# One attention loop on TensorE, a score mask built on the chip, and constants loaded in two parts

## The chip, the core and the metric

The kernel runs on one core of a Trainium2 chip. The metric is device time in microseconds (us). A core has five engines with instruction streams of their own: TensorE (PE, matmuls; its weight loads are listed as PEld), VectorE (DVE), ScalarE (ACT), GpSimd (POOL) and SyncE (SP, here the issuer of most DMAs). They meet only at semaphores.

## What is computed

Three stages, one after another: a decayed linear attention, a mixture of experts that sends each token to one of 8 experts, and a gated product with an output projection.

```python
def _attn_ref(q, k, v):                 # (4, 8, 768, 64) each
    gamma = 1.0 - 2.0 ** (-5.0 - np.arange(H))
    for t in range(S):
        state = gamma * state + einsum('bhd,bhe->bhde', k[:, :, t], v[:, :, t])
        y[:, :, t] = scale * einsum('bhd,bhde->bhe', q[:, :, t], state)

def _moe_ref(x, modality_id, w_gate, modality_bias, w1, w2):   # x: 3072 rows of 512
    logits = x @ w_gate + modality_bias[modality_id]
    e_idx = argmax(logits); gate_w = softmax(logits)[e_idx]
    out[mask] = gate_w[mask] * (relu(x[mask] @ w1[e]) @ w2[e])  # mask: rows of expert e

def _moe2_ref(x, w1, w2, w3, w_out):
    return ((x @ w1) * (x @ w2) @ w3) @ w_out
```

## The kernel before

The attention is cut into units: 6 chunks `c` of 128 positions by 4 batches `b`, 24 units in all, `u = 4c + b`. The state of a batch is carried from one chunk to the next, so unit `u` uses the state of unit `u - 4`. All four computing engines write their units out one after another in straight code (`each_unit`); there is no scheduler, so the order is the order in which the lines stand.

On PE a unit (`unit` in `block.tensor`) is five steps: `scores(u+1)`, the products of keys and queries of the *next* unit into banks 2 and 3; `from_state(u)`, what the old state contributes, into `attn`; `rows_and_logits(u-1)`, which turns the finished unit before into rows and multiplies by `w_gate`, into `pair`; `from_chunk(u)`, the masked scores by V, into `attn`; `update(u)`, the new keys by values, into banks 0 and 1. Chunk 0 has no `from_state` and chunk 5 no `update`. In the profile these are L749, L771, L762, L780 and L792.

The other engines follow. DVE, per unit: `masked(u)` multiplies the scores by the mask table `maskt` into `prob` (L981, two instructions); `keep_logits(u-2)` reduces the logits of two units ago out of `pair` (L987); `new_state(u-2)` (L999); `qdecay(u)`, which writes `qdk`, the decayed queries that `from_state(u)` reads (L991); in late units also a piece of weight preparation (L962). ACT, per unit and in this order: `keep(u-1)`, which waits for `s_lg`, that is for `keep_logits(u-1)`, and copies the rows out of `pair` to `x_keep`; then, after `from_chunk(u)`, the copy of `attn` to `xTu`, which signals `s_xTu` (both are L560, told apart by their tiles). POOL makes `kdk` for unit `u+2` when `update(u)` is done (L507). SP loads q, k transposed, v and k of each unit, 256 KB each, four units ahead, and stores `x_keep`.

`from_state(u)` waits for the copy of unit `u-1`, since both use `attn`; `scores(u+1)` waits for `masked(u)`, since banks 2 and 3 exist once; `rows_and_logits(u)` waits for `keep(u-1)`, since `pair` exists once.

At the start the mask table (512 KB) is SP's second transfer, and the table of small constants `small` (422 KB) is ACT's second. Behind the attention PE goes on with a product of `w3` and `w_out`, then with the experts' windows, then with the last stage, whose groups of 512 rows it already runs in an engine loop: `pe.Fori(1, NG - 1)`, four passes of one group.

Of the kernel before, what the change touches and what calls it, by code (L numbers as in the profile page):

```python
# [32 lines left out]
def build(nc, q_t, k_t, k, v, mod_id, w_gate, mod_bias, we1, we2, wa, wb, w3_t, w_out, out):  # L33
# [30 lines left out]
    lag = pos[None, :] - pos[:, None]  # L64
    mask_np = np.where(lag[:, None, :] >= 0, scale * gamma[None, :, None] ** np.maximum(lag, 0)[:, None, :], 0.0)
    half_head = lambda pair: gamma[2 * pair + (np.arange(P) // D)]
# [12 lines left out]
    c_mask = const("c_mask", mask_np.reshape(P, HP, 2, P).transpose(0, 2, 1, 3).reshape(P, H * P))  # L79
    c_qdec = const("c_qdec", qdec_np.reshape(P, HP * P))  # L80
    small_np = [("ident", np.eye(P)), ("before", before_np), ("ones", np.ones((P, P))), ("kdec", kdec_np.reshape(P, C * H)),
                ("grow", grow_np.reshape(P, C * HP)), ("segment", segment_np.reshape(P, E * NT)),
                ("erank", every(E - np.arange(E))), ("eidx", every(np.arange(E))),
# [14 lines left out]
    with ctx:  # L98
# [17 lines left out]
        sm = {n: small[:, a:a + w] for n, (a, w) in small_at.items()}  # L116
        ident = sm["ident"]
        iw = fixed("iw", [P, KD, XW])
        logits = fixed("logits", [P, E, NT])
# [29 lines left out]
        qdect = r("qdect", [P, HP, P])  # L149
        xTu = r("xTu", [P, KD, P])  # L150

# [31 lines left out]
        in_lane = r("in_lane", [P, NT, P])  # L183
        in_tile = r("in_tile", [P, NT, 2, NX])

        w_out_p = region(at_w + 32 * KB)("w_out_p", [P, 2, KF, DM], F32R)
# [45 lines left out]
        s_ldv = [sem(f"s_ldv{b}") for b in range(B)]  # L232
        s_mask = sem("s_mask")
        s_qk = sem("s_qk")
# [159 lines left out]
        def _(sp):  # L394
# [4 lines left out]
            def load(c, b, u):  # L399
                if c:  # L400
                    sp.wait_ge(s_up, u - B + 1)
                sp.dma_start(qkv[:, b, QT, :], slot_v[QT][b, c, :, :]).then_inc(s_ldq[b], 16)  # L402
                if u:
                    sp.dma_start(qkv[:, b, KT, :], slot_v[KT][b, c, :, :]).then_inc(s_ldq[b], 16)
                else:
                    sp.dma_start(maskt[:, :, :, :], c_mask.rearrange("p (r j t) -> p r j t", r=2, j=HP)).then_inc(s_mask, 16)
# [148 lines left out]
        def _(act):  # L555
            act.dma_start(qkv[:, 0, KT, :], slot_v[KT][0, 0, :, :]).then_inc(s_ldq[0], 16)
            act.dma_start(small[:, :], c_small).then_inc(s_const, 16)
            act.wait_ge(s_zero, 1)
            act.dma_start(iw[:, :, P:XW], w_gate.rearrange("(c p) e -> p c e", p=P)).then_inc(s_gatew, 16)
            copy = lambda o, i, **kw: act.activation(o, i, ACT.Copy, **kw)  # L560
# [19 lines left out]
            def unit(c, b, u):  # L580

                if u:
                    keep(u - 1)
                act.wait_ge(s_yTu, u + 1)
                copy(xTu[:, :, :], attn[:, :, 0:2 * P].rearrange("p r (m t) -> p r m t", m=2)).then_inc(s_xTu, 1)
# [7 lines left out]
            act.dma_start(mbias[:, :, :], mod_bias.unsqueeze(0).to_broadcast([P, NMOD, E])).then_inc(s_mod, 16)  # L593
            act.dma_start(mod_i[:, :, :], mod_id.bitcast(I32).rearrange("p (n two) -> p n two", two=2)).then_inc(s_mod, 16)
            each_unit(unit)
# [135 lines left out]
        def _(pe):  # L731
# [8 lines left out]

            def scores(c, b, u):
                pe.wait_ge(s_ldq[b], 32 * (c + 1))
# [9 lines left out]

            def rows_and_logits(u):
                pe.wait_ge(s_xTu, u + 1)
                if u:
                    pe.wait_ge(s_keep, u)
                else:
                    pe.wait_ge(s_gatew, 16)
                    pe.wait_ge(s_ident, KD)
                for j in range(KD):  # L760
                    for a in range(2):
                        i = pe.matmul(pair[halves(a), j, 0:XW], xTu[:, j, halves(a)], iw[:, j, :], start=True, stop=True, skip_group_check=True)  # L762
                i.then_inc(s_xl, 1)

            def from_state(b, u):
                pe.wait_ge(s_xTu, u)
                pe.wait_ge(s_qdk, u - B + 1)
                pe.wait_ge(s_state, u - B + 1)
                for j in range(HP):
# [4 lines left out]
            def from_chunk(c, b, u, first):  # L774
                pe.wait_ge(s_ldv[b], 16 * (c + 1))
                pe.wait_ge(s_prob, u + 1)
                for j in range(HP):
                    for r in range(2):
                        h = 2 * j + r
                        i = pe.matmul(attn[out_rows(j, r), r, j // 2 * P:(j // 2 + 1) * P], qkv[:, b, V, h * D:(h + 1) * D], prob[:, u % 2, r, j, :],  # L780
                                      start=(first and j < 2), stop=(j >= HP - 2), skip_group_check=True)
# [13 lines left out]

            def unit(c, b, u):
                if u + 1 < NT:
                    scores(c + (b + 1) // B, (b + 1) % B, u + 1)
                if c:
                    from_state(b, u)  # L800
                if u:
# [5 lines left out]
            scores(0, 0, 0)  # L807
            each_unit(unit)


# [14 lines left out]
            def counts():  # L825

                pe.wait_ge(s_const, 16)
                pe.wait_ge(s_one, 1)
                pe.wait_ge(s_keep, NT)
# [3 lines left out]

            w3_product(0, {2: lambda: rows_and_logits(NT - 1)})

# [103 lines left out]
        def _(dve):  # L939
# [61 lines left out]
            def unit(c, b, u):  # L1001
# [4 lines left out]
                if 1 < u <= NT - B + 1:  # L1006
                    if u == 2:
                        dve.wait_ge(s_const, 16)
                    new_state((u - 2) // B, (u - 2) % B, u - 2)
# [292 lines left out]
```

## Time and profile before

| | us |
|---|---|
| median of 3 runs (897.7 to 898.63) | 897.8 |
| the profiled execution | 897.12 |
| its span, first to last instruction | 895.4 |
| PE busy in it | 855.5 (96%) |
| DVE, ACT, POOL busy | 286.3, 238.5, 87.2 |

The profiled execution is 1.72 us longer than its span, and 0.68 us under the median. PE's share of busy time is an average over all stages: the attention takes roughly the first 112 us, and there PE has gaps that the later stages do not have. In the views below, "idle before" is the time an engine stood still before an instruction, with what ended it; "issue" means that the profile shows nothing that it waited for. PE's single-precision matmuls of the attention are listed as two passes each, so the eight matmuls of a step appear as x16 and the sixteen of `scores` as x32.

### The profile page before, as it was taken

To read this page: it belongs to the slowest core of one execution; us is meant where nothing else is said; L and a number is where in the kernel's file an instruction comes from. 1 tells how busy PE (TensorE), PEld (TensorE's weight loads), DVE (VectorE), ACT (ScalarE), POOL (GpSimd) and SP (SyncE) were. 2 spreads that over 40 slices of the span, in tenths; PEclk is the share of its full clock that TensorE was granted. 3 is DMA by queue.
4 is the path that set the end of the run, shared out by engine and by line. 5 is a ranking of instruction groups with operands and counts; after the bars stand their busy time and mean duration, and the time that the engine had idled before them with its cause. 6 is when DMAs were issued, how large, how long until landed. Compare 5 with 4: busy or idle time off the path is not lost.

```text
span 895.4 us, 14636 instructions
## 1 busy us (share of the span) xinstructions
PE 855.5 (96%) x5812; PEld 737.4 (82%) x5813; DVE 286.3 (32%) x495; ACT 238.5 (27%) x388; POOL 87.2 (10%) x110
## 2 busy tenths in 40 slices
PE   6989999998979999999998999999999999999995
PEld 5878878787979998888888788888888888888884
DVE  2658588531212334121416331221220230230210
ACT  1223423421212333121326322222231221231210
POOL 2222002202011020202000001001001001001001
PEclk9999999999999999999999999999999999999999
DMA  9999951323031252203054102002002002001000
GB/s 326 368 352 335 303 215 48 141 95 96 5 91 31 63 188 94 94 0 94 0 187 142 47 1 83 12 1 82 12 0 94 0 0 94 0 0 48 0 13 35
DMA packets 43484, 84.81 MB, mean 95 GB/s; under 512 B 7728, under 2 KB 7728, under 8 KB 43440
## 3 DMA queue, kind: packets, MB, share of 16 engines
q1 hardware_dynamic: 33376, 60.33, 19.6%
q0 software_dynamic: 4736, 14.72, 5.2%
q10 hardware_dynamic: 5328, 9.13, 3.1%
q8 instruction: 33, 0.54, 0.3%
q14 instruction: 11, 0.09, 0.0%
HBM read 63.16 MB, written 21.00 MB: 94 GB/s over the span
## 4 chain that ended last, share of the span: by engine, by line
PE 91%; issue 2%; DVE 2%; DMA 1%; SPq 1%; ACT 1%; ACTq 0%; POOL 0%; DVEq 0%
PE bank L387 47%; PE attn L387 33%; PE pair L762 3%; PE bank L749 2%; PE attn L780 2%; PE pair L842 1%; DMA qkv<-in_k_t_dram 1%; PE attn L771 1%; PE bank L792 1%; PE bank L894 1%; DVE we_p L962 0%; DVE w3T L962 0%; ACTq L342 0%; ACT we_p L560 0%; SPq L402 0%
## 5 line engine op out<-in xcount | busy, mean ns | idle before, releaser
L387 PE MATMUL bank<-yT,wab 128*128 128x512 f32 x1152 | 262.2, 389 | 1.7 <-issue 1.7
L387 PEld LDWEIGHTS bank<-yT,wab 128*128 128x128 f32 x1152 | 216.1, 188 | 46.7 <-issue 1.9
L387 PE MATMUL bank<-xT,we_p 128*128 128x512 f32 (+2 forms) x768 | 155.3, 364 | 11.5 <-issue 7.9
L387 PEld LDWEIGHTS bank<-xT,we_p 128*128 128x128 f32 x768 | 138.1, 195 | 28.3 <-issue 10.4
L387 PE MATMUL attn<-hT,we_p 128*128 128x512 f32 (+2 forms) x768 | 153.6, 357 | 0.0
L387 PEld LDWEIGHTS attn<-hT,we_p 128*128 128x128 f32 x768 | 132.9, 188 | 14.6
L387 PE MATMUL attn<-wc,gT 128*128 128x512 f32 x576 | 131.5, 389 | 0.0
L387 PEld LDWEIGHTS attn<-wc,gT 128*128 128x128 f32 x576 | 108.1, 188 | 22.5
L1242 DVE TENSOR_TENSOR g<-bank,acopy 128x512 f32<-128x512 f32 x48 | 33.2, 692 | 258.8 <-PE bank L387 258.8
L1203 DVE SCALAR_TENSOR_TENSOR hT<-bank,hT 128x512 fp32r<-128x512 f32 x64 | 44.1, 691 | 172.4 <-ACT hT L633 172.4
L633 ACT ACTIVATE hT<-bank 128x512 fp32r<-128x512 f32 x64 | 38.2, 598 | 114.9 <-PE bank L387 114.9
L560 ACT ACTIVATE gT<-g 128x512 fp32r<-128x512 f32 x48 | 30.3, 632 | 136.6 <-DVE g L1242 136.6
L548 POOL DMA_INDIRECT out_dram<-otile,row_id x24 | 23.2, 968 | 377.8 <-ACT otile L560 377.8
L560 ACT ACTIVATE yout<-attn 128x512 f32<-128x512 f32 x32 | 19.1, 597 | 114.6 <-PE attn L387 114.6
L560 ACT ACTIVATE acopy<-bank 128x512 f32<-128x512 f32 x48 | 28.7, 598 | 67.3 <-PE bank L387 67.3
L962 DVE TENSOR_TENSOR gT<-g,gT 128x512 fp32r<-128x512 f32 x48 | 33.3, 693 | 33.8 <-ACT gT L560 33.8
L560 ACT ACTIVATE otile<-attn,meta_in 128x512 f32<-128x512 f32 x24 | 16.6, 690 | 100.0 <-PE attn L387 100.0
L981 DVE TENSOR_TENSOR prob<-bank,maskt 128x512 f32<-128x512 f32 x48 | 30.8, 683 | 27.8 <-PE bank L749 21.1
L749 PE MATMUL bank<-qkv 64*64 64x128 f32 x768 | 28.4, 288 | 8.7 <-DMA qkv<-in_q_t_dram 4.4
L962 DVE TENSOR_TENSOR xT<-pair,xT 128x512 fp32r<-128x512 f32 x30 | 19.3, 686 | 54.1 <-ACT xT L560 53.9
L524 POOL DMA_INDIRECT xin<-x_rows,x_id x32 | 31.0, 969 | 11.1 <-issue 7.3
L560 ACT ACTIVATE x_keep<-pair 128x512 f32<-128x512 f32 x24 | 14.3, 598 | 63.6 <-DVE logits L987 63.6
(148 smaller groups left out, 559.7 us busy)
## 6 DMA issues: line engine op xcount, KB each, us to landing
we_raw<-in_moe_w_dram SPq DMA_DIRECT2D x6, 2048.0 KB, 9.1
yT_sorted<-yout ACTq DMA_DIRECT2D x8, 1024.0 KB, 4.9
qkv<-in_q_t_dram SPq DMA_DIRECT2D x24, 256.0 KB, 4.0
qkv<-in_v_dram SPq DMA_DIRECT2D x24, 256.0 KB, 6.0
x_rows<-x_keep SPq DMA_DIRECT2D x24, 256.0 KB, 5.7
ytile<-yT_sorted SPq DMA_DIRECT2D x6, 1024.0 KB, 5.1
qkv<-in_k_t_dram SPq DMA_DIRECT2D x23, 256.0 KB, 5.8
qkv<-in_k_dram SPq DMA_DIRECT2D x20, 256.0 KB, 6.5
```

The costliest lines, as they stand in the source:

```text
L387: i = pe.matmul(out_, left(a), right(b), start=(first and n == 0), stop=(last and n == 2), **kw)
L524: pool.indirect_dma_start(xin[:, t, :], None, x_rows[:, :], bass.IndirectOffsetOnAxis(ap=x_id[:, t:t + 1], axis=0)).then_inc(s_xin, 16)
L548: pool.indirect_dma_start(out[:, :], bass.IndirectOffsetOnAxis(ap=row_id[:, n:n + 1], axis=0), otile[:, n % 2, :], None).then_inc(s_out[n ...
L560: copy = lambda o, i, **kw: act.activation(o, i, ACT.Copy, **kw)
L633: act.activation(hT[:, HI, f, :], bank[f % 2][:, :], ACT.Relu).then_inc(s_hhi, 1)
L749: i = pe.matmul(bank[2 + r][halves(a), j * P:(j + 1) * P], qkv[head_rows(r), b, KT, keys], qkv[head_rows(r), b, QT, j * P:(j + 1) * P], st ...
L762: i = pe.matmul(pair[halves(a), j, 0:XW], xTu[:, j, halves(a)], iw[:, j, :], start=True, stop=True, skip_group_check=True)
L780: i = pe.matmul(attn[out_rows(j, r), r, j // 2 * P:(j // 2 + 1) * P], qkv[:, b, V, h * D:(h + 1) * D], prob[:, u % 2, r, j, :], start=(fir ...
L962: tt(pair(LO), raw, pair(HI).bitcast(F32), ALU.subtract).then_inc(sm_, 1)
L981: i = tt(prob[:, u % 2, r, :, :], bank[2 + r][:, :].rearrange("p (j t) -> p j t", j=HP), maskt[:, r, :, :], ALU.mult)
L1203: dve.scalar_tensor_tensor(hT[:, LO, f, :], bank[f % 2][:, :], 0.0, hT[:, HI, f, :].bitcast(F32), ALU.max, ALU.subtract).then_inc(s_hlo, 1)
L1242: tt(g32[:, f % 2, :], bank[2 + f % 2][:, :], acopy[:, f % 2, :], ALU.mult).then_inc(s_g, 1)
```

## The change

Five things change. PE's units of chunks 1 to 4 become one engine loop of four units that runs four times; chunks 0 and 5 stay as straight code. Inside a unit `from_chunk(u)` now stands ahead of `rows_and_logits(u-1)`, and `from_state`'s three waits (`s_xTu`, `s_qdk`, `s_state`) now stand ahead of `scores(u+1)`; `xTu` gets two buffers, since `rows_and_logits(u-1)` now runs while the copy of unit `u` may be due. The mask table is no longer loaded: PE multiplies a column of powers by a row of powers (`rank1`, 8 KB), and DVE multiplies the products by a triangle of ones. `small` is loaded in two parts: the identity, the strict triangle and `kdec` early, from ACT, the rest from SP with unit 1. The modality tables are issued in ACT's unit 2, the query table `qdect` with SP's unit 2, and `w_gate` comes laid out in one piece per partition. The orders of `unit` on DVE, ACT and POOL are the same as before, apart from those loads.

```diff
-                    sp.dma_start(maskt[:, :, :, :], c_mask...).then_inc(s_mask, 16)
...
                 if u == 1:
+                    sp.dma_start(small[:, first_w:], c_small[:, first_w:]).then_inc(s_rest, 16)
+                if u == 2:
                     sp.dma_start(qdect[:, :, :], c_qdec...).then_inc(s_tables, 16)
...
-            act.dma_start(small[:, :], c_small).then_inc(s_const, 16)
+            act.dma_start(rank1[:, :, :, :], c_rank1...).then_inc(s_rank1, 16)
+            act.dma_start(small[:, 0:first_w], c_small[:, 0:first_w]).then_inc(s_const, 16)
+            act.dma_start(iw[:, :, P:XW], w_gate...).then_inc(s_gatew, 16)
             act.wait_ge(s_zero, 1)
-            act.dma_start(iw[:, :, P:XW], w_gate...).then_inc(s_gatew, 16)
...
             def unit(c, b, u):      # ACT
+                if u == 2:
+                    act.dma_start(mbias[:, :, :], mod_bias...).then_inc(s_mod, 16)
+                    act.dma_start(mod_i[:, :, :], mod_id...).then_inc(s_mod, 16)
                 if u:
                     keep(u - 1)
                 act.wait_ge(s_yTu, u + 1)
-                copy(xTu[:, :, :], attn...).then_inc(s_xTu, 1)
+                copy(xTu[:, u % 2, :, :], attn...).then_inc(s_xTu, 1)
...
+            def mask_products():
+                pe.wait_ge(s_rank1, 16)
+                for r in range(2):
+                    for j in range(HP):
+                        h = 2 * j + r
+                        i = pe.matmul(bank[6 + r][:, j * P:(j + 1) * P], rank1[0:1, 0, h, :], rank1[0:1, 1, h, :], start=True, stop=True)
+                i.then_inc(s_outer, 1)
+
+            def scores(c, b, u, first=False, state_of=None):
+                pe.wait_ge(s_ldq[b], c * 32 + 32)
+                if not first:
                     pe.wait_ge(s_prob, u)
+                if state_of is not None:
+                    pe.wait_ge(s_xTu, u - 1)
+                    pe.wait_ge(s_qdk, state_of + 1)
+                    pe.wait_ge(s_state, state_of + 1)
+                pe.sem_inc(s_begun, 1)
...
-            def unit(c, b, u):
-                if u + 1 < NT:
-                    scores(c + (b + 1) // B, (b + 1) % B, u + 1)
-                if c:
-                    from_state(b, u)
-                if u:
-                    rows_and_logits(u - 1)
-                from_chunk(c, b, u, c == 0)
-                if c < C - 1:
-                    update(b, u, c == 0)
+            def unit(c, b, u, first=False, last=False):
+                if not (last and b == B - 1):
+                    scores(c + (b + 1) // B, (b + 1) % B, u + 1, state_of=None if first else (c - 1) * B + b)
+                elif last:
+                    pe.wait_ge(s_xTu, u)
...
+                if not first:
+                    from_state(b)
+                elif b:
+                    pe.wait_ge(s_xTu, u)
+                from_chunk(c, b, u, first)
+                if not (first and b == 0):
+                    rows_and_logits((b - 1) % B, u - 1, first and b == 1)
+                if not last:
+                    update(b, u, first)
...
+            mask_products()
+            scores(0, 0, 0, True)
+            for b in range(B):
+                unit(0, b, b, first=True)
+            with pe.Fori(0, C - 2) as past:
+                for b in range(B):
+                    unit(past + 1, b, past * B + (B + b))
+            for b in range(B):
+                unit(C - 1, b, (C - 1) * B + b, last=True)
...
-            dve.wait_ge(s_mask, 16)
+            dve.wait_ge(s_const, 16)
+            link(tt(tri[:, :], sm["before"], ident, ALU.add))
+            dve.wait_ge(s_outer, 1)
+            for r in range(2):
+                link(tt(maskt[:, r, :, :], bank[6 + r]..., tri..., ALU.mult))
             each_unit(unit)
```

On PE, one whole unit of chunk 1 in the kernel before, from `scores` to `update`, with the semaphores that each first matmul waits for:

```order
L749 MATMUL bank<-qkv 64x128 [waits s_prob,s_ldq2]
L749 MATMUL bank<-qkv 64x128 x15
L771 MATMUL attn<-qdk,state 64x128 [waits s_state,s_qdk,s_xTu]
L771 MATMUL attn<-qdk,state 64x128 x7
L762 MATMUL pair<-iw,xTu 64x136 [waits s_keep,s_xTu]
L762 MATMUL pair<-iw,xTu 64x136 x7
L780 MATMUL attn<-prob,qkv 64x128 [waits s_prob,s_ldv1]
L780 MATMUL attn<-prob,qkv 64x128 x7
L792 MATMUL bank<-qkv,kdk 64x64 [waits s_state,s_kdk]
L792 MATMUL bank<-qkv,kdk 64x64 x7
```

The wait for `s_xTu` of the finished unit stands behind `scores`. The same unit in the changed kernel, inside the loop (L770 is `scores`, L789 `from_state`, L798 `from_chunk`, L783 `rows_and_logits`, L810 `update`):

```order
L770 MATMUL bank<-qkv 64x128 [waits s_state,s_qdk,s_prob,s_xTu]
L770 MATMUL bank<-qkv 64x128 x15
L789 MATMUL attn<-qdk,state 64x128 x8
L798 MATMUL attn<-prob,qkv 64x128 [waits s_prob,s_ldv2]
L798 MATMUL attn<-prob,qkv 64x128 x7
L783 MATMUL pair<-iw,xTu 64x136 [waits s_keep,s_xTu]
L783 MATMUL pair<-iw,xTu 64x136 x7
L810 MATMUL bank<-qkv,kdk 64x64 [waits s_state,s_kdk]
L810 MATMUL bank<-qkv,kdk 64x64 x7
```

Three waits moved from `from_state` to `scores`, and the products into `pair` moved behind those of `prob`. On ACT the units stand as they did; this is its start in the changed kernel, up to the second unit:

```order
L562 DMA qkv<-in_k_t_dram 128x512
L563 DMA rank_102<-c_rank 1x2048
L564 DMA small<-c_small 128x304
L565 DMA iw<-in_moe_w_gate_dram 128x4x8
L567 ACT_TABLE_LOAD
L567 ACTIVATE act_warm<-zero 128x1 [waits s_zero]
L567 ACTIVATE xTu<-attn 128x512 [waits s_yTu]
L567 ACTIVATE x_keep<-pair 128x512 [waits s_lg]
L567 ACTIVATE xTu<-attn 128x512 [waits s_yTu]
L590 DMA mbias<-in_moe_modality_bias_dram 128x16
L591 DMA mod_i<-in_moe_modality_id_dram 128x48
```

The two modality loads moved from ahead of the first copy to behind the second; `x_keep` of a unit still stands ahead of `xTu` of the next.

## Rows read from the trace of the kernel before

**Rows 1.** Busy time by stretch: us, PE, PEld, DVE, ACT, POOL, clock, DMA share, GB/s

```profile
0.00:10.00 10.00, 1.98 (x32) 1.59 (x33) 1.31 (x3) 1.50 (x3) 2.33 (x10) 1.00 0.80 272
10.00:20.00 10.00, 9.29 (x184) 8.34 (x186) 3.33 (x7) 1.71 (x3) 2.20 (x3) 1.00 1.00 365
...
30.00:40.00 10.00, 8.02 (x184) 7.16 (x178) 6.08 (x16) 2.20 (x4) 2.08 (x2) 1.00 1.05 388
```

**Rows 2.** Chain that ended last, in order: start us, us, what; attention and its end

```profile
7.96 10.50 DMA qkv<-in_k_t_dram
18.51 1.10 PE bank L749 x32
...
22.03 1.03 PE bank L749 x32
...
25.48 1.17 PE bank L749 x32
...
30.75 1.04 issue
...
53.75 2.00 issue
...
99.24 1.03 PE bank L749 x32
...
102.66 1.03 PE bank L749 x32
...
110.15 1.58 PE bank L387 x6
111.74 1.10 PE pair L762 x16
```

**Rows 3.** Timeline of PE, one regular unit: start us, busy us, engine, line, instruction

```profile
91.86 1.10 PE L749 MATMUL bank<-qkv 64*64 64x128 f32 x32
...
92.79 0.62 PE L771 MATMUL attn<-qdk,state 64*64 64x128 f32 x16
...
93.34 1.15 PE L762 MATMUL pair<-iw,xTu 128*64 128x136 f32 x16
...
94.31 1.04 PE L780 MATMUL attn<-prob,qkv 128*64 128x128 f32 x16
...
95.19 0.64 PE L792 MATMUL bank<-qkv,kdk 128*64 128x64 f32 x16
...
95.75 1.10 PE L749 MATMUL bank<-qkv 64*64 64x128 f32 x32
```

**Rows 4.** Timeline, from rows_and_logits through DVE and ACT to PE; idle and releaser in brackets

```profile
106.89 0.60 ACT L560 ACTIVATE xTu<-attn 128x512 f32<-128x512 f32 x1
...
107.54 0.67 PE L771 MATMUL attn<-qdk,state 64*64 64x128 f32 x16 [0.70 <-ACT xTu L560]
...
108.13 1.15 PE L762 MATMUL pair<-iw,xTu 128*64 128x136 f32 x16
...
109.33 0.19 DVE L987 TENSOR_REDUCE logits<-pair 128x8 f32<-128x32 f32 x1 [0.60 <-PE pair L762]
109.55 0.60 ACT L560 ACTIVATE x_keep<-pair 128x512 f32<-128x512 f32 x1 [1.55 <-DVE logits L987]
```

**Rows 5.** Timeline of DVE, ACT and POOL in one regular unit

```profile
73.63 0.18 DVE L987 TENSOR_REDUCE logits<-pair 128x8 f32<-128x32 f32 x1
...
73.84 0.60 ACT L560 ACTIVATE x_keep<-pair 128x512 f32<-128x512 f32 x1 [2.28 <-DVE logits L987]
...
74.06 0.68 DVE L991 TENSOR_TENSOR qdk<-qkv,qdect 128x512 f32<-128x512 f32 x1
74.33 0.59 ACT L560 ACTIVATE xTu<-attn 128x512 f32<-128x512 f32 x1
```

**Rows 6.** Timeline of POOL and DVE where they overlap

```profile
67.03 1.04 POOL L507 TENSOR_TENSOR kdk<-qkv,small 128x512 f32<-128x512 f32 x1 [2.85 <-PE bank L792]
67.61 1.01 DVE L962 TENSOR_TENSOR w_out_p<-w_out_raw,w_out_p 128x512 fp32r<-128x512 f32 x1 [0.91 <-ACT w_out_p L560]
```

**Rows 7.** Timeline of the start

```profile
6.80 1.29 DVE L981 TENSOR_TENSOR prob<-bank,maskt 128x512 f32<-128x512 f32 x2 [6.68 <-DMA maskt<-c_mask]
7.26 1.00 POOL L498 COPY iw<-small 128x128 f32<-128x128 f32 x4 [6.31 <-DMA small<-c_small]
10.20 1.99 PE L749 MATMUL bank<-qkv 64*64 64x128 f32 x32 [3.79 <-DMA qkv<-in_k_t_dram]
```

**Rows 8.** Costliest groups, the loop of the last stage (busy, mean ns, idle before, releaser)

```profile
L387 PE MATMUL bank<-yT,wab 128*128 128x512 f32 x1152 | 262.2, 389 | 1.7 <-issue 1.7
```

**Rows 9.** Waits of PE from 200 to 260 us: total us, times, longest

```profile
PE bank L387 <- issue: 7.9, 2, 4.9
```

More of the change, by code:

```diff
@@ L64, in build @@
     lag = pos[None, :] - pos[:, None]
-    mask_np = np.where(lag[:, None, :] >= 0, scale * gamma[None, :, None] ** np.maximum(lag, 0)[:, None, :], 0.0)
+    rank1_np = np.stack([gamma[:, None] ** -pos[None, :], scale * gamma[:, None] ** pos[None, :]])
     half_head = lambda pair: gamma[2 * pair + (np.arange(P) // D)]
@@ L149, in build @@
         qdect = r("qdect", [P, HP, P])
-        xTu = r("xTu", [P, KD, P])
+        xTu = r("xTu", [P, 2, KD, P])
+        tri = r("tri", [P, P])
         x_keep = region(at_i)("x_keep", [P, NT, DM])
@@ L232, in build @@
         s_ldv = [sem(f"s_ldv{b}") for b in range(B)]
-        s_mask = sem("s_mask")
+        s_rank1 = sem("s_rank1")
+        s_outer = sem("s_outer")
+        s_rest = sem("s_rest")
+        s_begun = sem("s_begun")
         s_qk = sem("s_qk")
@@ L580, in unit @@
             def unit(c, b, u):
+                if u == 2:
+                    act.dma_start(mbias[:, :, :], mod_bias.unsqueeze(0).to_broadcast([P, NMOD, E])).then_inc(s_mod, 16)
+                    act.dma_start(mod_i[:, :, :], mod_id.bitcast(I32).rearrange("p (n two) -> p n two", two=2)).then_inc(s_mod, 16)
                 if u:
@@ L584, in unit @@
                 act.wait_ge(s_yTu, u + 1)
-                copy(xTu[:, :, :], attn[:, :, 0:2 * P].rearrange("p r (m t) -> p r m t", m=2)).then_inc(s_xTu, 1)
+                copy(xTu[:, u % 2, :, :], attn[:, :, 0:2 * P].rearrange("p r (m t) -> p r m t", m=2)).then_inc(s_xTu, 1)
                 if side_piece(u) is not None:
@@ L751, in scores, with rows_and_logits @@
                 i.then_inc(s_qk, 1)
-            def rows_and_logits(u):
+            def rows_and_logits(b, u, first=False):
                 pe.wait_ge(s_xTu, u + 1)
-                if u:
+                if not first:
                     pe.wait_ge(s_keep, u)
@@ L761, in rows_and_logits, with from_state @@
                     for a in range(2):
-                        i = pe.matmul(pair[halves(a), j, 0:XW], xTu[:, j, halves(a)], iw[:, j, :], start=True, stop=True, skip_group_check=True)
+                        i = pe.matmul(pair[halves(a), j, 0:XW], xTu[:, b % 2, j, halves(a)], iw[:, j, :], start=True, stop=True, skip_group_check=True)
                 i.then_inc(s_xl, 1)
[L765 to L768, printed above, removed]
+            def from_state(b):
                 for j in range(HP):
@@ L794, in update @@
                 i.then_inc(s_up, 1)
-            def unit(c, b, u):
-                if u + 1 < NT:
-                    scores(c + (b + 1) // B, (b + 1) % B, u + 1)
-                if c:
-                    from_state(b, u)
-                if u:
-                    rows_and_logits(u - 1)
-                from_chunk(c, b, u, c == 0)
-                if c < C - 1:
-                    update(b, u, c == 0)
-            scores(0, 0, 0)
-            each_unit(unit)
+            def unit(c, b, u, first=False, last=False):
[3 more added lines that the diff above has]
+                    pe.wait_ge(s_xTu, u)
+                    pe.wait_ge(s_qdk, (c - 1) * B + b + 1)
+                    pe.wait_ge(s_state, (c - 1) * B + b + 1)
+                if not first:
+                    from_state(b)
[15 more added lines that the diff above has]
+                unit(C - 1, b, (C - 1) * B + b, last=True)
             def w3_product(f, amid={}):
@@ L832, in counts @@
                 pe.matmul(bank[7][:, 0:E * NT], sm["ones"], chosen, start=True, stop=True).then_inc(s_cnt, 1)
-            w3_product(0, {2: lambda: rows_and_logits(NT - 1)})
+            w3_product(0, {2: lambda: rows_and_logits(B - 1, NT - 1)})
             def x_rows(w, chunks):
@@ L1283 @@
     swapped = place.reshape(-1)
-    laid["moe_w_gate"] = inputs["moe_w_gate"][swapped]
+    laid["moe_w_gate"] = inputs["moe_w_gate"][swapped].reshape(4, 128, -1).transpose(1, 0, 2).reshape(128, -1)
     laid["moe_w1"] = inputs["moe_w1"][:, swapped]
```

25 lines of the change are left out of this document (12 added, 13 removed).

## The prediction

> **What bounds the kernel now.** I read the busy time by stretch first, then the chain that ended last, then single units in the timeline. PE carries almost the whole span, so the question for each edit is whether PE waits more or less. In the attention it has gaps: 8.02 us busy in the ten from 30 to 40 [rows 1]. From the scores of unit 4 at 22.03 to those of unit 23 at 102.66 the chain runs for 80.63 us over 19 units [rows 2]. A regular unit takes 95.75 - 91.86 = 3.89 us, its five steps back to back [rows 3]; one without an update 102.66 - 99.24 = 3.42, the one of chunk 0 25.48 - 22.03 = 3.45 [rows 2]. So 16 x 3.89 + 2 x 3.42 + 3.45 = 72.5 us are PE's own work, and 8.1 us are gaps: five pieces called issue (the first and the longest in [rows 2]), with small gaps beside them. Ahead of that the start is set by transfers: the scores of unit 3, at 18.51, come 0.05 us after a K load that landed at 18.46 [rows 2].
>
> **The loop's gain.** If PE finds the loop's code in place on passes two to four, most of the 8.1 us go. Chunk 0, the first pass and chunk 5 still run code that PE meets for the first time, so I leave 1.0 us of gaps (bounds 0, and 3.1 for three pieces like the first). Loop-backs fall between an update and the scores, where PE will be waiting anyway (next part). Term: -8.1 + 1.0 = -7.1 us.
>
> The Trainium skill speaks against the loop in "Runtime: NRT & Kernel Launch", section "Instruction fetch mechanics": code is fetched ahead in sequence, and a taken branch to a target outside the window held forces a fetch, so unrolled code is preferred. The trace has a loop of this kind, the last stage's four passes of one group, and all its first products together stand idle for 1.7 us by issue [rows 8], so the row does not bear the rule out; by the row the sum stays, by the rule it becomes the third rival below.
>
> **The order and the moved waits: the largest term.** In the changed unit `scores(u+1)` waits for the copy `xTu(u-1)`. ACT's order is unchanged: ahead of that copy stands `keep(u-2)`, which waits for DVE's `keep_logits(u-2)`, which waits for `rows_and_logits(u-2)`. That step used to stand ahead of `from_chunk`, so its two followers were done by the time `from_chunk` ended. Now it stands behind it, so PE sends the products into `pair`, and what follows on DVE and ACT has only the update to hide behind. Let R be the start of `rows_and_logits`. From R to the logits' reduction 109.33 - 108.13 = 1.20 us, from there to `x_keep` 0.22 [rows 4], from `x_keep` to the copy behind it 74.33 - 73.84 = 0.49 [rows 5], from the copy's start to PE's first matmul 107.54 - 106.89 = 0.65 [rows 4]: 2.56 us from R to the next scores. From scores to R the steps keep their lengths in the new order: 92.79 - 91.86 = 0.93 for the scores, 0.55 for `from_state` (to the start at 93.34), 95.19 - 94.31 = 0.88 for `from_chunk` [rows 3]: 2.36 us. The unit therefore repeats every 2.36 + 2.56 = 4.92 us. No row shows what the five waits and the loop's register arithmetic ahead of `scores` add behind the last release. In the row with three such waits PE starts 0.05 us after the copy ends (106.89 + 0.60 to 107.54 [rows 4]), which lies in the 0.65; zero more is one bound, 0.35, seven times that, the other, and I take 0.08, near the row. So 5.0 us a unit, 1.11 over PE's work, in 16 units, and 1.58 over in the two without an update: 17.8 + 3.2 us. The first wait of the kind, ahead of the scores of unit 5, stands behind a unit without `from_state`: 0.93 + 0.96 + 2.56 = 4.45 for 3.45, 1.0 us more. Term: +22.0 us. Queued behind the waiting scores is all else of the unit; DVE's mask, SP's loads (after `update`) and POOL move with PE, so nothing of it is off the path.
>
> Behind the last scores nothing much changes: before, 111.74 - 102.66 = 9.08 us to the last `rows_and_logits` [rows 2]; after, 4.92 + 0.55 + 0.88 + 2.56 = 8.9, with six products in between as before. Term: -0.1 us.
>
> DVE could set the period instead of ACT. `qdk` starts 74.06 - 73.63 = 0.43 us behind the reduction and takes 0.68 [rows 5], so it ends at R + 1.20 + 0.43 + 0.68 = R + 2.31, under 2.56. But POOL's `kdk` now starts close by: the update starts 0.97 us after R, by the spacing of `rows_and_logits` to the next step, lasts 0.64 [rows 3], and POOL some 0.15 us later (an estimate from the regular units), R + 1.76, against R + 1.63 for `qdk`. Where POOL was first in this trace, DVE's product of two SBUF tiles took 1.01 us and ended 0.55 us after POOL did [rows 6]. Here DVE is first by 0.13 us, so I add nothing; the other order is a rival.
>
> The Trainium skill, "SBUF — State Buffer", section "Who interferes with whom", calls this an exclusive lock for the whole instruction, held by whichever starts first. The 1.01 us agree, and by that rule too DVE keeps its 0.68 us and the sum stays.
>
> **Start.** 512 KB of mask go from SP's queue ahead of the K load of unit 3; the rest of `small` and `qdect` still stand ahead of it. At 365 GB/s [rows 1] this is 1.4 us, at 272 GB/s 1.9; with the smaller `w_gate` pieces I take -1.5 us (bounds 0, where something else is as late, and -3.0, where the second part of `small` also slips behind). The mask costs PE 16 small passes, no more than an update's 0.64 us [rows 3], and DVE three operations, two of them like a mask product of 0.65 [rows 7]. Its inputs land before 7.26, when the whole of `small` had [rows 7], by some 2 us since they are 152 of 422 KB; the first mask product then starts near 7, as before at 6.80, and the scores that wait for it stood until 10.20 for a load [rows 7]. If that cover goes, up to 1 us is lost there, and the load of unit 3 hides it again. The two modality loads put about 1.2 us of issue on ACT in unit 2; `keep(1)` and `xTu(2)` are queued behind, and ACT idles 2.28 us before a regular `keep` [rows 5], so I cost them at nothing.
>
> **Sum.** -7.1 + 22.0 - 0.1 - 1.5 = +13.3 us. Against the profiled execution of 897.12 us this is 910.4; the median lies 0.68 above that execution, so the time I name is 911.0. What follows the attention moves with it.
>
> **Rivals.**
>
> *Faster: PE does not wait for the copy.* If something in the new order let `xTu` be ready when the update ends, a unit would stay at 3.89 us and the change would give 7.1 + 1.5 = 8.6 us: 889. The point from which it decides is the period: 18 units and the first must not pay more than 8.6 us, so 4.3 us a unit. For it speaks only that the second `xTu` buffer allows a copy while the rows are still being read; against it stands ACT's order, `keep` ahead of the copy, and four measured steps that sum to 2.56 us, where 1.53 (the update, 0.56 after 0.97) are covered. Chance 0.06, with 0.02 for a time within 0.2% (1.8 us, about what a measurement of this kernel can tell from no change).
>
> *POOL first.* If `kdk` takes the port before `qdk`, `qdk` ends at R + 1.76 + 1.04 + 0.55 = R + 3.35 and a unit takes 5.76 us, 0.76 more in 16 units: +12.2, so 923. The margin is 0.13 us. Chance 0.14.
>
> *Loop-backs fetch code.* PE's two entries into new branches cost 7.9 us, the longest 4.9, the other 3.0 [rows 9]. Three loop-backs at 3.0 to 4.9 us, less the 1.11 us of waiting that covers them: +5.7 to +11.4, so 917 to 922. Against it stands the 1.7 us of [rows 8]. Chance 0.06.
>
> *PE's clock falls.* The scores took 1.99 us at 10.20 [rows 7] and 1.10 later [rows 3], so at the lower of its two levels PE's 3.5 us of a period would grow by about 2.8, +50 in all: 961. PE would be busy 3.89 of 5.0 us, 78%; the stretch from 30 to 40 had 80% and a granted clock of 1.00 [rows 1]. Chance 0.04.
>
> **How the numbers follow.** The forecast has 0.68: its own ends are a period of 4.92 to 5.27 (-1.4, +4.9), gaps 0 to 3.1 (-1, +2.1) and a start of -3.0 to 0 (-1.5, +1.5), which do not all fall to one side: 907 to 918. The range adds the loop-backs, the near half of POOL first and some way down towards the gain: 905 to 922; out of it are the gain, the clock and half of POOL first, under 0.2. Faster 0.06, same 0.02, slower 0.92.
>
> **What would show it.** PE's waits should list `scores` on ACT's `xTu`, some 18 times, about 1.1 us each; scores should start 5.0 us apart; the issue pieces between 40 and 110 us should be gone; the mask's transfer too, and the first product of unit 3 should start near 17. `qdk` at 0.68 us says that DVE is first, at 1.5 that POOL is. Scores 3.9 us apart would prove the main term wrong.

## The result

The changed kernel takes 913.69 us (913.23 to 914.68, 4 runs) against 897.75 for the kernel before: a ratio of 1.0179, 95% interval 1.0161 to 1.0196. It is slower by 15.9 us; the forecast was 911.0 within 905 to 922, slower with a chance of 0.92.

The page of the changed kernel, its span and the busy times:

```profile
span 911.5 us, 14723 instructions
PE 857.0 (94%) x5828; PEld 738.9 (81%) x5829; DVE 289.2 (32%) x498; ACT 236.9 (26%) x388; POOL 91.7 (10%) x110
```

PE's busy time is almost the old one, so the time went into waiting. PE's waits in the first 150 us of the changed kernel (total us, times, longest):

```profile
PE bank L770 <- ACT xTu L567: 21.6, 19, 1.6
PE pair L754 <- DMA rank<-c_rank: 4.6, 1, 4.6
PE bank L770 <- issue: 1.8, 2, 1.5
PE attn L789 <- ACT xTu L567: 1.4, 1, 1.4
```

`scores` (L770) waits 19 times for ACT's copy, 1.1 us each. One unit of the changed kernel in the timeline shows the whole path, from `rows_and_logits` (L783) over the reduction (L1019), `x_keep` and `xTu` to the next scores:

```profile
56.16 1.10 PE L783 MATMUL pair<-iw,xTu 128*64 128x136 f32 x16
...
57.30 0.19 DVE L1019 TENSOR_REDUCE logits<-pair 128x8 f32<-128x32 f32 x1 [1.09 <-PE pair L783]
...
57.53 0.60 ACT L567 ACTIVATE x_keep<-pair 128x512 f32<-128x512 f32 x1 [4.11 <-DVE logits L1019]
57.74 0.68 DVE L1023 TENSOR_TENSOR qdk<-qkv,qdect 128x512 f32<-128x512 f32 x1
...
57.88 1.45 POOL L513 TENSOR_TENSOR kdk<-qkv,small 128x512 f32<-128x512 f32 x1 [3.75 <-PE bank L810]
58.02 0.59 ACT L567 ACTIVATE xTu<-attn 128x512 f32<-128x512 f32 x1
...
58.71 1.10 PE L770 MATMUL bank<-qkv 64*64 64x128 f32 x32 [0.99 <-ACT xTu L567]
```

From R = 56.16 to the scores it is 2.55 us; the sum made from [rows 4, 5] was 2.56. The pieces of the chain that ended last show how far the scores lie apart:

```profile
22.77 1.03 PE bank L770 x32
...
27.36 1.10 PE bank L770 x32
...
63.66 1.10 PE bank L770 x32
...
68.75 1.10 PE bank L770 x32
...
73.94 1.10 PE bank L770 x32
...
78.89 1.10 PE bank L770 x32
...
83.84 1.10 PE bank L770 x32
...
114.18 1.10 PE bank L770 x32
...
119.24 1.10 PE bank L770 x32
...
128.35 1.10 PE pair L783 x16
```

Inside a pass of the loop the distances are 5.09, 5.19, 4.95 and 4.95 us, 5.05 in the mean. The chain has 0.23 and 0.33 us by issue between the copy and the scores in the first two units of a pass and 0.09 in the other two; that the first two compute their wait values behind the release of the copy and the others ahead of it is a guess, since the profile does not list register instructions. The straight units of chunk 5, which have no such arithmetic, have 0.20 us there and lie 5.06 us apart, so on the whole the loop costs nothing here. The mean from unit 5 to unit 23 is (119.24 - 27.36) / 18 = 5.10 us, against 3.89 for a regular unit before [rows 3].

### The profile page after: what moved, and what is told of

The parts are those of the page before. It is cut to its first block, busy times and chain, and to the rows that moved or that the text cites. A ratio compares the mean times of both kernels' runs of the same rounds, so it can differ in the third digit from the quotient of the medians.

```text
span 911.5 us, 14723 instructions
## 1 busy us (share of the span) xinstructions
PE 857.0 (94%) x5828; PEld 738.9 (81%) x5829; DVE 289.2 (32%) x498; ACT 236.9 (26%) x388; POOL 91.7 (10%) x110
## 3 DMA queue, kind: packets, MB, share of 16 engines
q1 hardware_dynamic: 33376, 60.08, 19.3%
## 4 chain that ended last, share of the span: by engine, by line
PE 89%; DVE 3%; ACT 3%; issue 3%; ACTq 0%; DMA 0%; POOL 0%; DVEq 0%
PE bank L393 45%; PE attn L393 32%; PE bank L770 3%; PE attn L798 3%; PE pair L783 2%; PE pair L874 1%; ACT x_keep L567 1%; ACT xTu L567 1%; PE attn L789 1%; PE bank L926 1%; DVE logits L1019 0%; DVE we_p L994 0%; PE pair L754 0%; DMA rank<-c_rank 0%; DVE w3T L994 0%
## 5 line engine op out<-in xcount | busy, mean ns | idle before, releaser
L393 PEld LDWEIGHTS bank<-xT,we_p 128*128 128x128 f32 x768 | 136.2, 191 | 29.7 <-issue 11.3
L770 PE MATMUL bank<-qkv 64*64 64x128 f32 x768 | 28.5, 287 | 23.4 <-ACT xTu L567 21.6
L770 PEld LDWEIGHTS bank<-qkv 64*64 64x64 f32 x768 | 22.8, 140 | 26.7 <-issue 26.5
L567 ACT ACTIVATE otile<-attn,meta_in 128x512 f32<-128x512 f32 x24 | 16.6, 690 | 100.0 <-PE attn L393 100.0
L994 DVE TENSOR_TENSOR xT<-pair,xT 128x512 fp32r<-128x512 f32 x30 | 19.3, 686 | 54.1 <-ACT xT L567 53.9
```

What stands on the lines that cost most here:

```text
L393: i = pe.matmul(out_, left(a), right(b), start=(first and n == 0), stop=(last and n == 2), **kw)
L770: i = pe.matmul(bank[2 + r][halves(a), j * P:(j + 1) * P], qkv[head_rows(r), b, KT, keys], qkv[head_rows(r), b, QT, j * P:(j + 1) * P], st ...
L994: tt(pair(LO), raw, pair(HI).bitcast(F32), ALU.subtract).then_inc(sm_, 1)
```

## Experiments

Theory 1, from the prediction: two chains follow `rows_and_logits` before the next scores, ACT's `keep` and copy (2.56 us) and DVE's `qdk` (2.31 us), and only the update covers them. Rivals: the loop itself is the loss, or ACT's order alone. Each set of runs had the kernel before run beside it, at 895.5 to 895.8 us there, so times of different sets are compared by their ratio to it. The times in the expectations go by the kernel before at 897.75 us, some 2 us more than in these sets.

### The copy ahead of the keep

```diff
             def unit(c, b, u):      # ACT
-                if u:
-                    keep(u - 1)
                 act.wait_ge(s_yTu, u + 1)
                 copy(xTu[:, u % 2, :, :], attn...).then_inc(s_xTu, 1)
+                if u:
+                    keep(u - 1)
```

> The changed kernel with one edit: ACT copies attn to xTu ahead of the keep of the unit before. Changed kernel 913.7 us, scores 5.10 us apart in the mean. Theory 1 (two followers of rows_and_logits stand between it and the next scores: ACT's keep and copy at R+2.56, and DVE's qdk at R+2.31, R being the start of rows_and_logits): the copy is now hidden, but the scores still wait for qdk, so the period falls only to about 4.8, 18 x 0.3 = 5 us: about 908. Theory 2 (the loop with its register arithmetic is the loss): nothing moves, 913.7. Theory 3 (ACT's order alone is the loss): period 3.9 to 4.0, about 893.

Measured: 910.49 us, ratio 1.0162 (1.0127 to 1.0198). PE's waits of this kernel in the first 150 us:

```profile
PE bank L770 <- DVE qdk L1023: 10.3, 11, 1.5
PE bank L770 <- issue: 9.4, 10, 1.5
```

ACT is gone from the list and DVE's `qdk` stands in its place. "issue" is here very probably the same wait, put down by the profile to nothing, since those scores start 0.21 us behind the end of `qdk` (57.88 behind 57.67, 62.74 behind 62.53), and 0.15 us where the profile names it (67.55 behind 67.40):

```profile
56.99 0.68 DVE L1023 TENSOR_TENSOR qdk<-qkv,qdect 128x512 f32<-128x512 f32 x1
...
57.88 1.10 PE L770 MATMUL bank<-qkv 64*64 64x128 f32 x32 [0.91 <-issue]
```

By its time this kernel cannot be told from the changed one (1.0162 for 1.0179, within the interval), so the time does not decide between the theories; the trace does. In passes 2 to 4 the scores lie 4.80 to 4.87 us apart, as theory 1 said. The attention ends 3.5 us earlier in the trace (its `w3` product begins at 123.22 for 126.76), a little under the 5 expected, since unit 7 and the late units gain less. ACT's order alone is not the cause; it is one of two chains of nearly one length.

### The three waits back at from_state

```diff
             def scores(c, b, u, first=False, state_of=None):
...
-                if state_of is not None:
-                    pe.wait_ge(s_xTu, u - 1)
-                    pe.wait_ge(s_qdk, state_of + 1)
-                    pe.wait_ge(s_state, state_of + 1)
...
+            def from_state(c, b, u):
+                pe.wait_ge(s_xTu, u)
+                pe.wait_ge(s_qdk, (c - 1) * B + b + 1)
+                pe.wait_ge(s_state, (c - 1) * B + b + 1)
+                pe.sem_inc(s_begun, 1)
```

> The changed kernel with from_state's three waits (xTu, qdk, state) moved back from scores to from_state, behind a semaphore increment like that of scores; ACT's order and PE's order of steps stay. Theory 1: the copy still comes at R+2.56, but PE now has update and scores to do until R+1.53+0.93 = 2.46, so only 0.1 to 0.35 us a unit are exposed: period 4.05 to 4.25, 895 to 898 us. Theory 2 (loop): about 913. Theory 3 (ACT's order alone): the copy is as late as before and from_state waits for it instead, 910 or more.

Measured: 901.59 us, ratio 1.0067 (1.0046 to 1.0089). The chain that ended last in this kernel, scores and a gap of the first pass:

```profile
31.64 1.94 issue
...
60.98 1.03 PE bank L766 x32
...
65.11 1.03 PE bank L766 x32
...
69.33 1.03 PE bank L766 x32
```

A unit takes 4.12 to 4.26 us, within what was expected. The time is 4 us above the expected 895 to 898, by ratio 6: two gaps of 1.94 and 1.90 us in the first pass, of the kind seen before [rows 2], are back, now that PE does not stand waiting where they fall; the rest was not followed.

### rows_and_logits back ahead of from_chunk

```diff
-                from_chunk(c, b, u, first)
                 if not (first and b == 0):
                     rows_and_logits((b - 1) % B, u - 1, first and b == 1)
+                from_chunk(c, b, u, first)
```

> The changed kernel with rows_and_logits put back ahead of from_chunk; the waits stay at scores, ACT's order stays. Theory 1: the keep is done by the time from_chunk ends, so behind from_chunk there is the copy alone, 0.06 + 0.60 + 0.05 and some 0.15 of register work, against an update of 0.56: 0.3 us exposed, period about 4.2, about 897 us. Theory 2 (loop): 913. Theory 3 (ACT's order): keep still stands ahead of the copy, so 910 or more.

Measured: 901.51 us, ratio 1.0062 (1.0042 to 1.0083). PE's waits of this kernel, and two pieces of its chain, the scores ten units apart:

```profile
PE bank L770 <- ACT xTu L567: 8.3, 19, 0.9
```

```profile
50.17 1.10 PE bank L770 x32
...
93.35 1.10 PE bank L770 x32
```

The copy is still the last to come, but by 8.3 us in all for 21.6; units take 4.24 to 4.49 us, mean (93.35 - 50.17) / 10 = 4.32, for some 4.2 expected. The time missed the expected 897 by 4.5 us: 0.12 a unit is some 2 of them, and the two units around DVE's preparation of the bias tables take 45.69 - 35.66 = 10.03 us, 1.4 over two others. ACT's order is that of the changed kernel in this run and in the one ahead of it, so the rival that it alone is the loss falls: each of PE's two edits costs little by itself, the order alone 0.3 us a unit over 3.89 (the run ahead of this one), the moved waits alone 0.4 (this run); together they cost 1.2.

### The loop written out

```diff
-            with pe.Fori(0, C - 2) as past:
-                for b in range(B):
-                    unit(past + 1, b, past * B + (B + b))
+            for c in range(1, C - 1):
+                for b in range(B):
+                    unit(c, b, c * B + b)
```

> The changed kernel with the loop of chunks 1 to 4 written out as straight code, all else the same. Theory 1: PE waits for the copy as before, period 5.06 as in the straight chunk 5 now, and code that is met for the first time adds gaps, part of which the waits hide: 913 to 919 us. Theory 2 (the loop is the loss, code in place the gain): the loss of some 22 us goes and the gaps of 8 come back: about 899.

Measured: 914.87 us, ratio 1.0217 (1.0194 to 1.024). PE's waits of this kernel:

```profile
PE bank L770 <- ACT xTu L567: 22.1, 19, 1.6
```

The waits are the same, so the loop is not the loss. And no gap by issue like those before (0.94 us and more) comes back although all code of the attention is straight again: its `w3` product begins at 126.97, for 126.76 with the loop. The scores lie 5.06 us apart here too. The trace also shows what the instruction queue that differs with PE's code (q8 in the DMA view) moved: nothing between 50 and 110 us with the loop, nine blocks of code, 0.02 MB each, without it. So in this order the loop saves nine fetches of code, which lie under the waits, and 0.2 us of the attention. By ratio the straight form is 0.4% slower (1.0217 for 1.0179); where that would lie the two traces, with spans of 911.8 and 911.5 us, do not show.

### What the loop is worth without the waits

Both PE edits undone, once with the loop and once as straight code; the mask is made on the chip in both:

```diff
-                from_chunk(c, b, u, first)
                 if not (first and b == 0):
                     rows_and_logits((b - 1) % B, u - 1, first and b == 1)
+                from_chunk(c, b, u, first)
...
-                    pe.wait_ge(s_xTu, u - 1)      # the three waits again at from_state
...
-            with pe.Fori(0, C - 2) as past:       # only in the straight form
+            for c in range(1, C - 1):
...
```

> The changed kernel with both PE edits undone inside the loop (rows_and_logits ahead of from_chunk, the three waits at from_state behind a semaphore increment), so the loop, the mask on the chip and the two-part constants remain. Theory 1 (order and waits are the whole loss): period 3.9 to 4.1, few gaps, the start 0.7 us later than before: 892 to 895 us against 897.75. Theory 2 (register arithmetic in the loop costs as much as it saves): 897 or more.

> As the kernel with both PE edits undone, but with chunks 1 to 4 as straight code: of the change there remain the mask on the chip and the constants. Theory 1: the kernel before with its gaps of 8 us and a start 0.7 us later, 898 to 899 us; its distance to the looped form is what the loop is worth without the waits, 3 to 6 us. Theory 2 (loop worth nothing): the same time as the looped form.

Measured: 895.86 us with the loop, ratio 0.9993 (0.9976 to 1.001); 903.11 as straight code, 1.0083 (1.0061 to 1.0105). The loop is worth 7.2 us here, more than the 3 to 6 expected, and both times lie above the expected ones (892 to 895, 898 to 899). In the chain of the looped form the units of passes 2 to 4 follow without a gap, and the product behind the attention begins at 108.86; in that of the straight form it begins at 114.31, so 5.4 of the 7.2 us lie in the attention:

```profile
51.96 1.03 PE bank L766 x32
...
55.85 1.03 PE bank L766 x32
...
59.74 1.03 PE bank L766 x32
...
108.86 1.58 PE bank L393 x6
```

```profile
26.19 1.41 issue
...
38.47 2.41 issue
...
62.51 1.48 issue
...
86.07 1.36 issue
...
114.31 1.59 PE bank L393 x6
```

The first fence is the looped form, the second the straight one. At 3.89 us a unit the register arithmetic of the loop does not show. From 50 to 100 us the instruction queue moved no block in the looped form and eight in the straight one, and each of the straight form's six gaps (the four shown, 0.75 at 32.74 and 0.82 at 79.57) begins within some 2 us behind such a block. That goes with fetching as their cause; it does not show why seven other blocks from 25 to 100 us brought no gap.

### The mask loaded again

The changed kernel with the mask from memory, and the looped form of the old PE order with it:

```diff
+                    sp.dma_start(maskt[:, :, :, :], c_mask...).then_inc(s_outer, 16)   # SP, second transfer
...
-            act.dma_start(rank1[:, :, :, :], c_rank1...).then_inc(s_rank1, 16)
...
-            mask_products()
...
-            link(tt(tri[:, :], sm["before"], ident, ALU.add))
-            dve.wait_ge(s_outer, 1)
-            for r in range(2):
-                link(tt(maskt[:, r, :, :], bank[6 + r]..., tri..., ALU.mult))
+            dve.wait_ge(s_outer, 16)
```

> The changed kernel with the mask table loaded again by SP as second transfer, without the products of powers on PE and their multiplication on DVE; constants still in two parts. Theory 1 (the start of the changed kernel is 2.2 us later than forecast because the mask's inputs land at 8.4 us and 16 passes of 0.24 us run ahead of the first scores): the mask lands near 6.8 as before, the scores of unit 4 start near 21.3 in place of 22.8, about 912.3 us. Rival (the start is set by the K loads in either form): the 512 KB come back ahead of them and nothing is gained, 913.7 or up to 915.

> As the kernel with both PE edits undone inside the loop, and the mask table loaded as before, so the loop and the two-part constants remain of the change. Theory 1: another 1.4 us less than with the mask made on the chip, 891 to 894 us. Rival for the start (K loads set it): the same as with the mask made on the chip, or up to 1 us more.

> The kernel of old PE order, loop and loaded mask, beside the shifted one on the same chip: 0.9916 of the kernel before as in its first run, about 7.5 us less.

Measured: 906.49 us, ratio 1.0113 (1.0092 to 1.0134), for the changed kernel with the loaded mask; 887.88, ratio 0.9916 (0.9893 to 0.9939), and in the second run 887.97, ratio 0.9902 (0.9882 to 0.9921), for the looped old order with it. The last is the one form faster than both kernels, by 0.8 to 1.0% than the one before.

The gain of some 6 us (1.0179 to 1.0113) is four times what was expected; in the old order it is 8.0 (895.86 to 887.88). The start of the changed kernel shows where the expected part lies:

```profile
4.59 3.78 PE L754 MATMUL pair<-rank 1*128 1x128 f32 x16 [4.59 <-DMA rank<-c_rank]
...
8.30 1.99 PE L770 MATMUL bank<-qkv 64*64 64x128 f32 x32
8.51 0.29 DVE L1056 TENSOR_TENSOR tri<-small 128x128 f32<-128x128 f32 x1 [8.38 <-DMA small<-c_small]
...
8.83 1.42 DVE L1059 TENSOR_TENSOR maskt<-pair,tri 128x512 f32<-128x512 f32 x2
...
10.42 1.29 DVE L1013 TENSOR_TENSOR prob<-bank,maskt 128x512 f32<-128x512 f32 x2 [0.17 <-PE bank L770]
11.81 1.99 PE L770 MATMUL bank<-qkv 64*64 64x128 f32 x32 [1.53 <-issue]
```

The products of powers take 3.78 us, 0.24 a pass, ahead of the first scores, and the first part of `small`, though it is a third of the table, lands at 8.5 us, behind the 7.26 of the whole table before [rows 7]. The second scores start at 11.81 for 10.20. With the loaded mask the scores of unit 4 start at 21.07 for 22.77, and the product behind the attention 1.9 us earlier. The other 4 us lie in the experts' stage, and the next experiment shows what most of them hang on.

### The code moved by 33 instructions

```diff
+            for _ in range(33):
+                pe.sem_inc(s_begun, 1)
             scores(0, 0, 0, True)
```

> The kernel of old PE order, loop and loaded mask with 33 semaphore increments on PE ahead of its first scores, where it waits 4.4 us for a load anyway; nobody waits on them. They stand where the 32 instructions of the mask's products stand in the changed kernel, so all later code lies at the place that it has there. Theory 1 (the gap of 5 us at the end of the experts' first window and the 1.4 us near 480 us hang on where the code lies): both come back, 6 us more than the same kernel without them. Rival (they hang on the mask's work or the transfers of the start): at most 1 us more.

Measured, on the looped old order with the loaded mask: 893.57 us, ratio 0.9976 (0.996 to 0.9992), 5.6 us more than the same kernel without the increments beside it. The chain of the shifted form at the experts' first window and at the end of it:

```profile
210.34 2.65 issue
248.32 4.43 issue
```

The unshifted form has one of the two, and in the other's place 0.29 us in its first run, shown here, and 0.20 in its second:

```profile
208.21 2.36 issue
245.92 0.29 issue
```

By its place, behind the 192 products of the first window, the second gap is where PE branches over code that it has not run. It stands in the kernel before too, with 4.87 us, and in the changed kernel with 5.12; in all, eleven of the thirteen kernels have it, with 4.2 to 5.2 us, and the two without it, the changed and the old order with the loop and the loaded mask and no increments, have 0.2 to 0.3 in three traces. The DMA view ties it to fetched code: in each of the eleven traces that instruction queue moved one block of 0.02 MB inside the gap, and in the three others none in the 5 us from the same place on. There the last block had come ahead of the branch (at about 247 for 249.34 in the second run of the unshifted form).

The gap costs more than its length: behind it the granted clock of the shifted form is 0.50, the lower of its two levels, from 252.8 to 254.8, and the next 96 products take 18.34 us; in the unshifted form beside it the clock is 1.00 there and they take 16.91. Together this is 5.7 us. The rest of the distance nearly cancels: with the increments the product behind the attention begins 1.4 us later (108.90 for 107.54), but the first window ends 1.0 earlier (248.32 for 249.34), since in that run of the unshifted form the first gap was the longer one (3.48 us), with a clock of 0.53 to 0.76 in the 4.6 us behind it.

So most of what the mask seemed to cost beyond the start is the place of later code, moved by the 32 instructions of its products: with the loaded mask the changed kernel has 0.30 for its 5.12 us. The gap of 1.4 us near 480 us did not come back, so that half of the expectation was wrong.

### POOL first

Two tries at the rival in which `kdk` takes the shared port ahead of `qdk`: one small DVE copy ahead of `qdk`, then three.

```diff
+                    for a in (tmax, tsum, gate):     # the first try: tmax alone
+                        dve.tensor_copy(a[:, :], sm["ones"][:, 0:NT])
                     qdecay(c, b)
```

> The changed kernel with one small DVE copy (128x24, some 0.17 us) ahead of qdk in chunks 1 to 5, so that POOL's kdk, at R+1.76, starts before qdk, at R+1.8, in place of behind it. If the two exclude each other and the first keeps the other out: qdk ends 0.55 us behind kdk, at R+3.35, the unit repeats every 5.75 us in the 16 units with a kdk, and the kernel takes about 924 us. If they only slow each other a little: qdk ends by R+2.6, ACT's copy stays the last to come, 914 us.

> As with one small DVE copy ahead of qdk, which moved it by 0.08 us only and left it 0.05 us ahead of POOL's kdk; now three copies into three tiles, so qdk comes near R+1.9, behind kdk's R+1.76. If the first keeps the other out: qdk ends near R+3.35, the 16 units with a kdk repeat every 5.7 us, scores wait for qdk instead of the copy, about 924 us. If they share: qdk ends by R+2.7, 0.15 us over the copy, 916 us at most.

The first try gave 914.44 us, ratio 1.0196 (1.0168 to 1.0224), and decided nothing: the copy ran into `qdk`'s start and delayed it by 0.08 us only, so DVE was still first by 0.05. The second gave 937.71, ratio 1.0462 (1.0442 to 1.0483). Its timeline:

```profile
70.81 1.10 POOL L513 TENSOR_TENSOR kdk<-qkv,small 128x512 f32<-128x512 f32 x1 [6.49 <-PE bank L810]
...
70.91 1.54 DVE L1023 TENSOR_TENSOR qdk<-qkv,qdect 128x512 f32<-128x512 f32 x1
...
72.66 1.10 PE L770 MATMUL bank<-qkv 64*64 64x128 f32 x32 [2.01 <-issue]
```

`qdk` starts 0.10 us behind `kdk`, takes 1.54 us instead of 0.68 and ends 0.54 after `kdk`, the 0.55 read from [rows 6]. The price was right; the time is 13.7 us above the 924 expected, mostly since a second rival came with it, the clock. The busy times of two stretches of this kernel, with the granted clock ahead of the last two columns:

```profile
80.00:90.00 10.00, 8.05 (x163) 7.34 (x156) 5.77 (x13) 1.75 (x4) 1.10 (x1) 0.88 0.72 215
...
100.00:110.00 10.00, 8.05 (x164) 7.44 (x158) 5.43 (x12) 1.60 (x3) 1.10 (x1) 0.83 0.70 218
```

The mean granted clock of these stretches is 0.88 and 0.83 of its higher level, so parts of them run at the lower one; PE stands 2.0 us in each unit there, and six units with the lower clock in them take 7.5 us instead of 5.9, some 9.7 us in all. In the changed kernel, with 1.1 us in each unit, it is 1.00 in every ten us from 20 to 120.

## The prediction, point by point

- **The moved waits and the order, +22.0 us: right, and a little too small.** From unit 4's scores to unit 23's the trace has 96.47 us for 80.63: +15.8 us, where the terms +22.0 and -7.1 made +14.9. Of the period, 2.55 us from R stand for 2.56. What the waits and the register arithmetic add behind the release, taken at 0.08, came to 0.13 in the mean of a pass (5.05 for 4.92); since the straight form has the same period, 5.06, it is not the arithmetic of the loop. The rest of 5.10 is for the most part some 0.4 us at unit 7, where DVE's preparation of the bias tables delays the next mask. That 18 units pay it was right (19 waits of 21.6 us). That DVE's chain was close behind ACT's was right too: it took over at 4.83 us when the copy moved forward.
- **The loop's gain, -7.1 us: it came, but it cannot be credited to the loop.** The gaps went, and the code was in place: no instruction block moved in passes 2 to 4. But the straight form of the same order, with nine blocks, does not have the gaps either: PE's wait of 1.1 us a unit hides them. Either cause is enough alone, so beside the waits the loop was worth 0.2 us of the attention. That -7.1 fits the sum is thus in part luck: it was argued from the loop, and the waits alone would have given it. The loop's own worth, 7.2 us, appears only where the waits are gone.
- **Loop-backs fetch code: did not happen.** Passes 2 to 4 run at 3.89 us a unit in the looped old order, with no instruction block moved. The Trainium skill's rule on branches ("Runtime: NRT & Kernel Launch", "Instruction fetch mechanics") does not show at these loop-backs. It agrees with the forward branch at the end of the experts' first window, where eleven traces have a gap of 4.2 to 5.2 us with one block inside it, and three have neither. Why 33 instructions at the front decide on it was not settled.
- **PE's clock falls: did not happen in the changed kernel, and did with POOL first.** The 1.99 us of the scores at 10.20 were taken for the lower level, but the granted clock there reads 1.00 [rows 1], so that row did not show it. Scores at the lower level take up to 1.89 us in the second try (113.06), near the price taken.
- **The start, -1.5 us: the step that failed.** Unit 4's scores start at 22.77 for 22.03, so it was +0.7. Two things were mis-sized: PE's 16 passes, taken for at most an update's 0.64 us, took 3.78; and the inputs, taken to land 2 us ahead of 7.26, landed at 8.5. The cover named for it, the wait of the second scores until 10.20, was too short: they now start at 11.81, behind the first mask product (10.42 + 1.29), so the mask came onto the path. Each of the two would have been enough: the first scores end at 10.29 and the mask is made at 10.25. The K load of unit 3 did not hide it again, as the prediction had it: that unit's scores start at 19.3, where they were to start near 17.
- **POOL first: did not happen.** `qdk` stood 0.14 us ahead of `kdk` (57.74 and 57.88; forecast 0.13), kept its 0.68 us, and `kdk` took 1.45 us instead of 1.04. The second try shows that the price of the other order was real. The Trainium skill's rule ("SBUF — State Buffer", "Who interferes with whom") agrees in both directions: whichever started second took longer, `kdk` 1.45 us here and `qdk` 1.54 in the second try.
- **The end, -0.1 us: right.** 9.11 us from unit 23's scores to the last `rows_and_logits`, for 9.08.
- **The sum:** +0.7 + 15.8 + 0 = 16.6 us at the end of the attention, and 0.5 us won back behind it: the span grew by 16.1, the medians by 15.9, forecast 13.3.

## To carry to other kernels

Before a wait is moved ahead of a step, or a step behind another, follow what the *other* engines do between the step's end and the wait's release, in their own order: here a moved wait that costs 0.4 us a unit by itself and a moved step that costs 0.3 cost 1.2 together. A gap that vanishes with a change need not have been removed by the part that was meant to: take that part out and see whether the gap returns. And a table that is cheap in bytes can be dear in the passes and waits that make it, if they stand ahead of everything else.

## What the runs showed of the hardware that I had not expected

- 33 instructions at the front of PE's program bring a gap of 4.43 us into the experts' stage, 240 us later, that is 0.2 to 0.3 without them; one instruction block of 0.02 MB moves inside the gap, and the products behind it run at a granted clock of 0.50 for 2 us and more and cost another 1.4 us. Two forms of a kernel that differ only in early code can so differ by 5 us there.
- A loop of four units moved no instruction block in its passes 2 to 4, where the same code written out moved eight in 50 us, with gaps of 0.8 to 1.5 us behind three of them.
- A matmul pass of the mask (1*128) takes 0.24 us where a pass of the scores right behind it (64*64) takes 1.99 / 32 = 0.06, at a granted clock of 1.00 in both stretches. The two differ in rows and in columns of weights; which of them makes the price is not shown.
- A DVE product of two SBUF tiles that starts 0.10 us behind a POOL product loses 0.86 us (1.54 for 0.68); one that starts 0.05 us ahead loses nothing, and POOL loses 0.4 to 0.5 (1.45 to 1.53 for 1.04).
- The granted clock fell in the second try of POOL first, where PE stood for 2.0 us in each unit of 5.9, with no gap longer than that; in the kernel before it stayed at 1.00 beside a gap of the same length that came singly (2.00 us at 53.75 [rows 2], with 1.00 from 50 to 60).
